# First mixture of a fused attention and two-mixture kernel: a and b by seven half products per pair of token blocks, y summed in SBUF

## The reference, cut to what matters

```python
attn = softmax(q, over d) @ (softmax(k, over s).T @ v)   # 4 batches, 8 heads, 576 tokens, 64 wide
x = attn as [2304 tokens, 512]
a = x @ w1; b = x @ w2                                   # [2304, 1024]
y = (a * b) @ w3 @ w_out                                 # [2304, 512]
p = probs / (sum(probs) + 1e-9)                          # 4 experts
out = sum over e of p[:, e] * (relu(y @ W1[e]) @ W2[e])  # [2304, 512]
```

## Time and profile before

| | us |
|---|---|
| runs, median (lowest, highest) | 1160.54 (1160.22, 1160.78) |
| the profiled execution | 1160.11 |
| its span, first to last instruction | 1158.1 |
| PE busy | 1139.9, 98% |
| DVE, ACT, POOL busy | 586.5, 289.9, 285.3 |
| first matmul of the first mixture at | 94.77 |
| first matmul of the experts at | 399.84 |

### The profile page before, as it was taken

The page is one execution under the profiler, slowest core; times in us unless marked ns, Lnnn a source line. Parts: engine busy times, 40 slices in busy tenths (PEclk is TensorE's granted clock), DMA queues, the critical chain, the costliest instruction groups (busy, mean ns, idle before and its releaser), DMA issues.

```text
span 1158.1 us, 16259 instructions
## 1 busy us (share of the span) xinstructions
PE 1139.9 (98%) x6304; PEld 1047.9 (90%) x6304; DVE 586.5 (51%) x878; ACT 289.9 (25%) x588; POOL 285.3 (25%) x350
## 2 busy tenths in 40 slices
PE   9999999999999899999999999999999999999998
PEld 7778999999999888989999989999998999999997
DVE  6974321212212965555555555555555555555555
ACT  5664221212212332112222111222221112222111
POOL 1574000000004024132242231322422314224210
PEclk9999999999999999999999999999999999999999
DMA  9741100000001000010010000100100001001012
GB/s 363 251 169 61 50 1 1 0 0 0 0 0 37 0 1 30 8 36 18 19 36 10 26 19 17 36 18 18 36 0 36 18 18 37 18 18 36 1 55 109
DMA packets 12590, 46.58 MB, mean 40 GB/s; under 512 B 1552, under 2 KB 1552, under 8 KB 11536
## 3 DMA queue, kind: packets, MB, share of 16 engines
q1 hardware_dynamic: 12560, 46.18, 11.2%
HBM read 41.46 MB, written 4.72 MB: 40 GB/s over the span
## 4 chain that ended last, share of the span: by engine, by line
PE 93%; DVE 4%; ACT 1%; issue 1%; DVEq 0%; ACTq 0%
PE b_ring L1016 9%; PE b_ring L1017 9%; PE b_ring L1015 9%; PE b_w L1015 7%; PE b_w L1017 7%; PE b_w L1016 7%; PE b_kv L1017 5%; PE b_kv L1016 5%; PE b_kv L1015 5%; PE b_w3t L1015 5%; PE b_w3t L1017 5%; PE b_w3t L1016 5%; PE b_kmax L1015 4%; PE b_kmax L1017 4%; PE b_kmax L1016 4%
## 5 line engine op out<-in xcount | busy, mean ns | idle before, releaser
L976 DVE SCALAR_TENSOR_TENSOR acc<-b_ring,pg,acc 128x512 f32<-128x512 f32 x180 | 135.1, 751 | 109.5 <-PE b_ring L1017 109.5
L1016 PE MATMUL b_ring<-u,hT 128*128 128x512 f32 x384 | 149.7, 390 | 0.0
L1017 PE MATMUL b_ring<-u,hT 128*128 128x512 f32 x384 | 149.6, 390 | 0.0
L1015 PE MATMUL b_ring<-u,hT 128*128 128x512 f32 x384 | 149.4, 389 | 0.0
L595 ACT ACTIVATE hT<-b_w 128x384 fp32r<-128x384 f32 x72 | 35.4, 492 | 449.6 <-DVE b_w L954 445.4
L380 POOL TENSOR_SCALAR uf<-stage 128x256 fp32r<-128x256 f32 x48 | 19.6, 408 | 332.3 <-PE b_w L1017 216.7
L976 DVE SCALAR_TENSOR_TENSOR acc<-b_kv,pg,acc 128x512 f32<-128x512 f32 x90 | 67.6, 751 | 60.0 <-PE b_kv L1017 59.9
L1016 PEld LDWEIGHTS b_ring<-u,hT 128*128 128x128 f32 x384 | 72.1, 188 | 15.6
L1015 PEld LDWEIGHTS b_ring<-u,hT 128*128 128x128 f32 x384 | 72.1, 188 | 15.4
L1017 PEld LDWEIGHTS b_ring<-u,hT 128*128 128x128 f32 x384 | 72.1, 188 | 15.1
L1017 PE MATMUL b_kv<-u,hT 128*128 128x512 f32 x192 | 75.5, 393 | 0.0
(11 more groups left out here) (185 smaller groups left out, 2728.8 us busy)
## 6 DMA issues: line engine op xcount, KB each, us to landing
stage<-in_exp_w SPq DMA_DIRECT2D x32, 512.0 KB, 3.2
kT<-in_k SPq DMA_DIRECT2D x4, 1152.0 KB, 8.7
qb<-in_q SPq DMA_DIRECT2D x6, 768.0 KB, 9.1
out<-acc SPq DMA_DIRECT2D x18, 256.0 KB, 2.0
stage<-in_moe_w3t SPq DMA_DIRECT2D x8, 512.0 KB, 5.7
vb<-in_v SPq DMA_DIRECT2D x4, 1024.0 KB, 8.8
stage<-in_moe_w SPq DMA_DIRECT2D x8, 512.0 KB, 3.6
wraw<-in_moe_w_out SPq DMA_DIRECT2D x4, 512.0 KB, 6.4
```

Source lines behind the costliest of these rows:

```text
L976: nc.vector.scalar_tensor_tensor(acc[:, tile, :], O_BANK[t % TT], scale, acc[:, tile, :], ALU.mult, ALU.add).then_inc(acc_added, 1)
L1015: nc.tensor.matmul(ps, w_hi_, x_hi_, start=start, stop=False, skip_group_check=onto)
L1016: nc.tensor.matmul(ps, w_hi_, x_lo_, start=False, stop=False, skip_group_check=onto)
L1017: return nc.tensor.matmul(ps, w_lo_, x_hi_, start=False, stop=stop, skip_group_check=onto)
```

## The change

Only the first mixture, its preparation and the hand-over to the experts are rebuilt; the experts' arithmetic stays.

- A "unit" is one m of 8 by one pair of 3 (`UNITS`, 24 units). The 2 x 2 weight matrix is (columns of w1, columns of w2) by (first, second half of the 512 features); the result's first row is a, its second b, for both blocks of the pair. PE forms it by the same seven products as in the experts: 42 matmuls of 384 columns instead of 48.
- The order of a unit's products is spread over two slots (`mix_slot(n)`: A11 of n, A22 and S4 of n-1, S2 and A12 of n, y of n-1, S1 and S3 of n).
- y is no longer summed over m in PSUM. `mix_out` forms 8 tiles of 3 matmuls per unit in a ring of three banks, and DVE adds each to `whole` in SBUF (`mix_add`, 8 per unit; for the first m a copy).
- DVE forms a in two halves from PSUM and a snapshot (`a_first`, `a_second`); ACT takes three snapshots of 128 x 384 per unit.
- x is copied whole by ACT (`x_part`) and split later, with the sums, into seven forms `xf` of 128 x 768 per pair: high parts on ACT (`form_hi`), sums and the low parts of T1 to T4 on DVE (`t_form`, `form_lo`), the low parts of B11, B21, B22 on POOL. The same is done again with y for the experts. W is copied whole too; POOL splits one piece per m (`mix_rows`), and POOL makes the weights' sums and forms for each m as it does for the experts.
- The first forms may be written only when W is finished (`room_for_x_forms`), since they lie where its operands lay.

The core of the diff:

```diff
-    xy = [at("xy_hi", [P, NB, KD, TB], F32R, XY), at("xy_lo", [P, NB, KD, TB], F32R, XY + 36864)]
+    xf = [at(f"xf{i}", [P, 7, 2, 2, TB], F32R, FORMS + i * 43008) for i in range(NPB)]
+    whole = [at(f"whole{i}", [P, 2, KD, TB], F32, ACC + i * 12288) for i in range(NPB)]
...
+            def mix_add(n, t0, t1):
+                m, pb = UNITS[n]
+                if t0 == 0 and m:
+                    dve.wait_ge(mix_added, MIX_TILES * (max(p for p in range(n) if UNITS[p][1] == pb) + 1))
+                for t in range(t0, t1):
+                    half, d = t // KD, t % KD
+                    dve.wait_ge(mix_ready, MIX_TILES * n + t + 1)
+                    to, ps = whole[pb][:, half, d, :], O_BANK[t % TT][:, 0:TB]
+                    if m:
+                        nc.vector.tensor_tensor(to, ps, to, ALU.add).then_inc(mix_added, 1)
+                    else:
+                        nc.vector.tensor_copy(to, ps).then_inc(mix_added, 1)
+
+            def mix_slot(n, ahead=True):
+                c22_part(n)
+                gate(n - 1, 0)
+                a_second(n - 1)
+                gate(n - 1, 1)
+                gate_lo(n - 1, 0)
+                gate_lo(n - 1, 1)
+                if ahead:
+                    a_first(n)
+                mix_add(n - 1, 0, MIX_TILES)
...
-            def mlp_y(i):
-                for c in range(KF):
-                    pe.wait_ge(g_split, i * KF + (c + 1))
-                    for d in range(KD):
-                        last = three(bank[4 + d][:, 0:TB], wf[HI][:, c, d * P:(d + 1) * P], wf[LO][:, c, d * P:(d + 1) * P],
-                                     g[:, c, HI, :], g[:, c, LO, :], c == 0, c == KF - 1)
+            def mix_out(n, t0, t1):
+                m, pb = UNITS[n]
+                hi, lo = wf_of(m)
+                for t in range(t0, t1):
+                    half, d = t // KD, t % KD
...
+                    if t % KD == 0:
+                        pe.wait_ge(g_lo, 2 * n + half + 1)
+                    if MIX_TILES * n + t >= TT:
+                        pe.wait_ge(mix_added, MIX_TILES * n + t + 1 - TT)
...
+                    three(O_BANK[t % TT][:, 0:TB], hi[:, d * P:(d + 1) * P], lo[:, d * P:(d + 1) * P],
+                          g[:, HI, half, :], g[:, LO, half, :], True, True).then_inc(mix_ready, 1)
+
+            def mix_slot(n):
+                mix_a11(n)
+                mix_a22(n - 1)
+                mix_s4(n - 1)
+                mix_s2(n)
+                mix_a12(n)
+                mix_out(n - 1, 0, MIX_TILES)
+                mix_s1(n)
+                mix_s3(n)
```

More of the change, by code:

```diff
@@ new lines, in _ @@
+            weight_sums(KF)
+            weight_form(KF, A11)
+            weight_form(KF, S2)
+            form_lo(3, B11)
+            weight_form(KF, A12)
+            form_lo(3, B21)
+            weight_form(KF, S1)
+            weight_form(KF, S3)
+            form_lo(3, B22)
+            weight_form(KF, A22)
+            weight_form(KF, S4)
+            form_lo(4, B11)
+            form_lo(4, B21)
+            form_lo(4, B22)
+            pool.wait_ge(mix_ready, MIX_TILES * NM)
+            u2_rows(0)
@@ L494, in _, with slot @@
+            def slot(e, par):
+                slot_begin(e, par)
+                relu_c11(e)
             w3t_part(0)
@@ L650, in _ @@
             for s in range(1, 2 * NPB):
-                slot(NU - 2 * NPB + s, s % 2)
-            slot(NU, 0, ahead=False)
+                slot(NE - 2 * NPB + s, s % 2)
+            slot_begin(NE, 0, ahead=False)
         @block.vector
@@ L979, in begin_c @@
-            def begin_c(n):
-                c11_part(n + 1)
-                relu_lo(B11, 0, 0, Y_BANK, n + 1)
-            begin_c(0)
-            finish_c(1, 1)
-            for form in (T1, T2, T3):
-                t_lo(NPB - 1, form)
-            add_out(1, 0, 0, True)
+            mix_add(0, 0, 8)
+            a_first(1)
+            form_lo(1, T4)
+            form_lo(2, T1)
+            c22_part(2)
+            form_lo(2, T2)
+            gate(1, 0)
+            a_second(1)
+            gate(1, 1)
@@ new lines, in _ @@
+            gate_lo(1, 0)
+            form_lo(2, T3)
+            mix_add(1, 0, 2)
+            gate_lo(1, 1)
+            mix_add(1, 2, 8)
+            a_first(2)
+            form_lo(2, T4)
+            for n in range(3, NM - 1):
+                mix_slot(n)
+                if n == 4:
+                    shares()
+            for form in (T1, T2, T3, T4):
+                t_form(3, form)
+            mix_slot(NM - 1)
+            for form in (T2, T1, T3):
+                form_lo(3, form)
@@ new lines, in _ @@
+            for n in range(3, NM):
+                mix_slot(n)
+            operands(0, 0, A11, B11)
+            product(uf, A11, B11, 0, X_BANK[0], True)
+            mix_a22(NM - 1)
+            mix_s4(NM - 1)
+            operands(0, 0, S2, T2)
+            pe.wait_ge(snapped[0], NM + 1)
+            product(uf, S2, T2, 0, X_BANK[0], False)
+            operands(0, 0, A12, B21)
+            pe.wait_ge(c11_ready, NM)
+            product(uf, A12, B21, 0, Y_BANK, True)
+            mix_out(NM - 1, 0, MIX_TILES)
```

1298 lines of the change are left out of this document (667 added, 631 removed).

## The result

The changed kernel takes **1167.22 us** (median of 5 runs, 1164.39 to 1167.94) beside 1160.54 (5 runs, 1160.22 to 1161.01) of the kernel before. The ratio is 1.0054, 95% interval 1.0043 to 1.0065: **slower by 0.5%**, where 1147.4 was forecast. It lies outside the range too, on the side of the rival in which the lock decides (1164.4). The profiled execution took 1167.2, of which the span is 1165.2.

What follows compares the result with a forecast made beforehand. PE, busy for 98% of the span, was taken as the bound. 1160.1 - 24.9 + 3.8 + 7.7 - 1.5 + 1.8 = 1147.0, and 0.4 more for the median gave 1147.4 us, range 1137 to 1162.

Steps and rivals of the forecast that it cites:

- the rival in which the lock decides: Head and hand-over: DVE loses each turn to POOL, costing 15 and +10; 1164.4 us in all, chance 12%.
- Term 1, the matmuls: First mixture: 66 matmuls per unit instead of 72, 144 fewer over 24 units, -24.9 us.
- Term 2, the ring: Steady slots: the fourth tile of y waits for its bank, 0.16 us a slot, +3.8 us over 24 slots.
- the rival of whole durations: Steady slots: DVE's additions run at 0.59 us each, losing 0.72 a slot, 17.3 in all; 1160.9 us, chance 6%.
- Before W ends: Ahead of W's end: DVE loses splits of x and W, part of PE's idling goes; -1.5 us, ends -4 and +2.
- Term 3, the head: Behind W's end: PE waits as DVE's and POOL's two-input SBUF work takes turns; +7.7 us, ends 0 and 15.
- The five stalls: Head: PE waits for `kv_scale` 2.6, S2 of unit 0 1.3, A11 of unit 1 2.2, S4 of unit 0 2.1, S2 of unit 1 3.2.
- In the last three: Head: A11 of unit 1, S4 of unit 0, S2 of unit 1, each behind a whole POOL instruction; half taken, 3.8 us.
- Term 4, the hand-over: From first mixture to experts: DVE's late forms and lost locks cost 9.5 us, +1.8 over before, ends -5 and +8.

Runs made afterwards that it cites:

- e12: Changed kernel with `a_first` of a steady slot behind the eight additions instead of ahead of them (19 slots); 1165.43 us.
- e1: Changed kernel without POOL's 18 low parts of B11, B21 and B22 in the first mixture, so part of the computation is missing; 1152.81 us.
- e8: Changed kernel with 54 extra matmuls on PE, results unread, in two waits of the head and one ahead of S4 of unit 23; 1162.61 us.
- e4: Changed kernel with ACT's two snapshots of the second expert slot ahead of the high parts of T3 and T4 of pair 1; 1161.20 us.
- e5: Changed kernel with DVE's, ACT's and POOL's queues reordered at the hand-over, one low part moved from DVE to POOL; 1156.42 us.
- e6: Changed kernel with DVE's and ACT's queues reordered in the head, four low parts of B forms moved from POOL to DVE; 1161.54 us.
- e7: Changed kernel with the edits of e5 and e6 together; 1150.87 us, ratio 0.9921 to the kernel before.

## Why the prediction was wrong

It was made against a profiled execution and missed by 1167.2 - 1147.0 = 20.2 us. By its steps:

- **Term 1, the matmuls: right.** 6160 of them, PE never idle in the steady part.
- **Term 2, the ring: right.** Slot 11.58 forecast, 11.605 measured, with the one stall at the fourth tile (0.15 against 0.16), and e12 takes it away. DVE's eight additions of such a slot take 4.07 in all, 0.50 apart, so the rival of whole durations is out.
- **Before W ends: -1.5 forecast, -4.0 measured** (idle 3.9 up to the last `kv` against 7.9 in the earlier trace rows), the low end of that term.
- **Term 3, the head: the failed step.** Without a wait the head would last about 33.9 (e1's 37.19 less its waits of 3.3), so it lost 16.8 and 3.0 ahead of it: 19.8 against 7.7, outside even the upper end of 15. The five stalls are there with 2.98, 4.10, 1.41, 4.02 and 0.71 us, 13.2 in all, and the term failed in three steps:
  - The low clock behind these waits was put at nothing, without a reason given in this term. It took some 5.4 us (the two windows above), and e8 got 2.0 to 4.1 back. This is the largest single part.
  - S2 of unit 0 was charged 1.3 and waited 4.10. It was priced behind ACT's high parts and four sums, with no turn of POOL among them, and two of the sums lasted 2.58 and 2.36.
  - "In the last three DVE loses the lock each time, which need not be; I take half of them": 3.8 where 6.1 were measured. Taken in full they were 7.5, so here the halving cost 2.4 us. The places were right, the single sizes were not (2.2, 2.1 and 3.2 against 1.41, 4.02 and 0.71).
- **Term 4, the hand-over: failed too.** A loss of 21.4 (91.14 - 69.7) against 9.5 forecast: waits of 14.6 (1.06, 2.92, 6.32, 2.18 and 2.07) and some 5.7 of low clock. Two steps: "What I do not charge is a lower clock, since none of these gaps is near the 5.2 us" was false, since one gap was 6.32 and spells of 0.32 a step follow the waits of 2.92 and 2.18 too. And the walk through DVE's queue left out ACT's, where the snapshots stood behind high parts that wait for DVE (6.32; e4). Here e5 gives back 10.3 by order, with one low part moved to POOL, and e1 1.8 without POOL's low parts. What the rest of POOL's passes cost there no run shows.
- The deviations sum to 0.6 - 2.5 + 12.1 + 11.9 = 22.1 against 20.2; the times "without a wait" are no better than that.
- **The rival.** "The lock decides" named the sign and, for the head, the mechanism, and its 15 + 10 was nearer than the forecast. Its 1164.4 is near the 1167.2 in part by luck: it charged the lock alone, and some 11 us of the measured loss are the low clock. It got 12% because a single row of one POOL pass (1.6 lost) was read as the usual case, and because "most POOL passes wait for ACT". They do, but DVE waits for ACT too: ACT's copy of x released DVE's queue at 110.10 and its high part POOL's three at 110.81, so both ran at once.

The Trainium skill (SBUF — State Buffer, Who interferes with whom) says that whoever issues first holds the shared ports for the whole instruction and the other one blocks. The trace agrees (2.57 for 0.95). That the two engines then take turns is what the rows show.

What stays open: how much of e6's remaining 10 us is capacity and how much is an order not yet found, what POOL's passes cost at the hand-over, and why the runs of the changed kernel spread over 3.5 us where those of the kernel before spread over 0.8. For the last e4 has a hint: its three runs at a mean granted clock of 0.987 or 0.988 took 1163.94 to 1164.77, its seven at 0.990 or 0.991 1158.85 to 1161.91.

## What to carry to other kernels

Work out the instructions that read two SBUF tensors on DVE and on POOL as one queue, each by its whole duration and in turns, and only then ask what PE waits for; don't halve a wait because it need not happen. A stage that PE could only just feed has no cover for the work of a saving made elsewhere: here 24.9 us less of matmuls in 24 slots put 24 passes of DVE and 9 of POOL in front of the first three. Put what PE waits for ahead of what only fills in, on every queue between (ACT's too). Give waits of some 2 us or more a range for the clock: nothing, or 1.5 us for a spell of 3.4 and up to 3 for one of 6.8.

## What the runs showed of the hardware

- DVE and POOL take turns when both have two-input SBUF work queued: three DVE instructions in a row lasted 2.55 to 2.59 instead of 0.95 beside three of POOL's in 6.92. A wait for a row of w2 cost a DVE low part the same way (3.01, e1). DVE's instructions with one PSUM input did not pay it (0.55 to 0.57 in the steady slots of the kernel after, with POOL busy for 76 us of 210).
- The granted clock fell behind waits much shorter than the 5.24 of the earlier trace rows: 2.18, 2.92, 4.02 and 4.10 in the kernel after. The length of the wait alone doesn't decide it. The kernel after kept 1.00 behind 2.98 (window 89 to 101), and e6, e8 and e12 kept it behind 2.29. At 2.07 the kernel after kept it, e4 lost it behind 2.06. At 1.68 e6 kept it and e7 lost it (105 to 110: 1.00 and 0.66).
- The slow spell lasted 3.5 us at 394.85 and over 6 us in the head, where PE worked through all of 105 to 110 at 0.67.
- 54 matmuls that nobody reads, put into three such waits, made the kernel 4.6 us faster (e8).
